# Strided sparse attention and a rational MLP on one core: TensorE turns x, and q, k and P of the first two batches

## The reference

```python
scores = scale * np.matmul(q, k.transpose(0, 1, 3, 2))
mask_local = (rel >= 0) & (rel < stride)
mask_strided = (rel >= 0) & (pos[None, :] % stride == pos[:, None] % stride)
...
attn = softmax(np.where(masks, scores, -1e9))      # the first 4 heads local, the last 4 strided
x = (attn @ v).transpose(0, 2, 1, 3).reshape(B * S, H * D)
h = x @ w_in                                       # 512 -> 2048
P = a[0] + a[1] * h + a[2] * h**2 + a[3] * h**3
Q = 1.0 + np.abs(b[0]) * np.abs(h) + np.abs(b[1]) * h**2
out = (P / (Q + 1e-06)) @ w_out                    # 2048 -> 512
```

## Time and profile before

| | us |
|---|---|
| median of 3 runs | 518.57 (515.09 to 522.15) |
| the profiled execution | 515.17 |
| its span, first to last instruction | 513.4 |

### The profile page before, as it was taken

One profiled execution on the slowest core, in us unless ns is written; L12 is line 12 of the kernel. 1 busy time (PEld: TensorE's weight loads), 2 busy tenths in 40 slices (PEclk: granted clock), 3 DMA queues, 4 the chain that ended last, 5 costly groups with the idle time before them and its releaser, 6 DMA issues.

```text
span 513.4 us, 7637 instructions
## 1 busy us (share of the span) xinstructions
PE 360.7 (70%) x3328; PEld 166.3 (32%) x3328; DVE 343.0 (67%) x286; ACT 272.9 (53%) x249; POOL 63.8 (12%) x104
## 2 busy tenths in 40 slices
PE   0024312678288979985977859997997898888980
PEld 0002110333133444532533325443442343333330
DVE  2001220138738988929959939996999999989940
ACT  0002000228338758581667556947968978788540
POOL 4022000200201100300401400030010010100010
PEclk9999999999558979997989969997999999998996
DMA  8989966997959969996899995472125110110111
GB/s 146 198 162 147 184 120 114 151 139 147 156 103 165 178 142 175 172 145 150 165 210 143 165 206 90 96 134 49 40 65 96 41 42 20 41 42 19 44 58 44
DMA packets 138769, 60.39 MB, mean 118 GB/s; under 512 B 128048, under 2 KB 134704, under 8 KB 138096
## 3 DMA queue, kind: packets, MB, share of 16 engines
q1 hardware_dynamic: 128560, 32.11, 36.9%
q0 software_dynamic: 10176, 27.80, 27.1%
HBM read 40.47 MB, written 23.59 MB: 125 GB/s over the span
## 4 chain that ended last, share of the span: by engine, by line
PE 33%; DMA 21%; ACT 16%; DVE 15%; SPq 8%; issue 5%; POOL 0%; DVEq 0%; POOLq 0%
PE ps_h L669 15%; PE ps_out L715 10%; DMA ptL<-pL 6%; ACT u L693 6%; DMA xt<-xL 5%; DMA ptS<-pS 4%; ACT u L691 4%; DMA tq<-q 4%; ACT h L673 3%; SPq L441 3%; SPq L643 2%; DVE u L690 2%; DVE z L696 2%; DVE h L700 2%; PE ps_s L715 2%
## 5 line engine op out<-in xcount | busy, mean ns | idle before, releaser
L669 PE MATMUL ps_h<-xt,Win 128*128 128x512 bf16 x576 | 152.4, 409 | 23.9 <-ACT h L673 16.5
L673 ACT ACTIVATE h<-ps_h 128x512 bf16<-128x512 f32 x144 | 104.9, 743 | 66.7 <-PE ps_h L669 62.5
L715 PE MATMUL ps_out<-Wout,h 128*128 128x512 bf16 x512 | 125.2, 396 | 6.1 <-ACT os L720 6.1
L669 PEld LDWEIGHTS ps_h<-xt,Win 128*128 128x128 bf16 x576 | 53.6, 103 | 104.3 <-ACT h L673 36.6
L715 PEld LDWEIGHTS ps_out<-Wout,h 128*128 128x128 bf16 x512 | 50.1, 101 | 69.5 <-ACT os L720 8.6
L691 ACT ACTIVATE u<-u,consts 128x4096 bf16<-128x4096 bf16 x18 | 66.5, 3695 | 5.6 <-DVE u L690 5.6
L693 ACT ACTIVATE u<-u 128x4096 bf16<-128x4096 bf16 x18 | 65.1, 3619 | 0.0
L726 POOL DMA_DIRECT2D out_dram<-os x36 | 25.8, 715 | 287.0 <-ACT os L720 287.0
L489 PE MATMUL ps_s<-ML,IDN 128*128 128x480 bf16 x32 | 10.8, 425 | 48.5 <-DMA tk<-tk 48.3
L508 DVE TENSOR_REDUCE ng<-ps_s 128x10 bf16<-128x960 f32 x16 | 18.3, 1142 | 37.6 <-PE ps_s L498 37.6
L700 DVE TENSOR_TENSOR h<-z,u 128x4096 bf16<-128x4096 bf16 x18 | 41.0, 2280 | 1.5 <-ACT u L693 1.4
(11 more groups left out here) (43 smaller groups left out, 305.7 us busy)
## 6 DMA issues: line engine op xcount, KB each, us to landing
out_dram<-os POOLq DMA_DIRECT2D x36, 256.0 KB, 2.5
q<-in_q_dram POOLq DMA_DIRECT2D x16, 288.0 KB, 6.7
k<-in_k_dram POOLq DMA_DIRECT2D x16, 288.0 KB, 9.1
vL<-v SPq DMA_DIRECT2D x32, 96.0 KB, 3.0
v<-in_v_dram POOLq DMA_DIRECT2D x8, 288.0 KB, 7.5
vS<-in_v_dram POOLq DMA_DIRECT2D x16, 144.0 KB, 11.6
xs<-xS SPq DMA_DIRECT2D x16, 144.0 KB
Win<-in_moe_w_in_dram POOLq DMA_DIRECT2D x4, 512.0 KB, 16.5
```

Source lines behind the costliest of these rows:

```text
L669: r = e.matmul(ph.t[:, :], Win[:, kk, f * 128:(f + 1) * 128], xt.t[:, kk, :], start=(kk == 0), stop=(kk == NK1 - 1))
L673: P.op("act", lambda e, f=f, ph=ph, h=h: e.activation(h.t[:, f % G, :].rearrange("p (j c k) -> p j k c", k=2, c=32), ph.t[:, :].rearrange( ...
L715: r = e.matmul(pot, groups[g].t[:, j, m * 128:(m + 1) * 128], Wout[:, kk, :], start=(kk == 0), stop=(kk == NF - 1))
```

## The change

PE turns x in all batches: the tokens of xS and xL are transposed in the bank `sm`, and ACT copies them in token order into a circular buffer `XT` of three chunks, in two passes of 128 columns for each kind (`turn`); the DMA transposes and the DRAM copy of xS go. As x is in token order now, the copy of h is written without the stride. In the first two batches POOL loads q and k straight into tiles of the h ring (`stage`), in 96 partitions, and PE transposes them, and P, into PSUM; ACT and DVE copy them out (`loads_pe`, `trp`). Batch 1's transposes of q and k wait for the fourth tile of the first chunk's MLP (`early`). Win comes in two column halves with a tile each, eight loads in all; batch 1's loads and Wout no longer wait for batch 0. A small ACT copy at the start brings the table load there. The planner counts POOL as free from 5 us on. Lines of the diff that only rename or that repeat a pattern are left out.

```diff
--- before.py
+++ after.py
@@ -103,7 +103,7 @@
                 d.users.append(o)
         pend = {e: [] for e in self.ENG}
         avail = {e: [] for e in self.ENG}
-        free = {e: 0.0 for e in self.ENG}
+        free = {e: 5.0 if e == "pool" else 0.0 for e in self.ENG}
         order = {e: [] for e in self.ENG}
         dmafree = {e: 0.0 for e in self.ENG}
         for o in self.ops:
@@ -260,6 +260,9 @@
     NBK = 8
     SB = S // 16
     NR = 64 + SB
+    TP = 96
+    TW = S * D // TP
+    NPE = 2
 
...
-    xs = nc.dram_tensor("xs16", [B, S, HL * D], bf)
     T_q = [[Tile(f"q{b}{n}") for n in "LS"] for b in range(B)]
     T_k = [[Tile(f"k{b}{n}") for n in "LS"] for b in range(B)]
     T_v = [Tile(f"v{b}") for b in range(B)]
...
     Win = sb("Win", [128, NK1, Fmid])
     Wout = sb("Wout", [128, NF, Fout])
-    T_win = Tile("win")
+    T_win = [Tile(f"win{i}") for i in range(2)]
     T_wout = Tile("wout")
     ML = sb("ML", [128, NR2 * KW])
     MS = sb("MS", [128, NBK * SB])
...
-    R_xt = ring("xt", 3, [128, NK1, CH])
+    XT = sb("XT", [128, NK1, 3 * CH])
+    T_xt = [Tile(f"xt{i}") for i in range(3)]
...
+    T_wm = Tile("warm")
+    WM = sb("WM", [128, 2], f32)
+    P.op("dve", lambda e: e.memset(WM[:, :], 1.0), 0.1, -2e6, m=[T_wm])
+    P.op("act", lambda e: e.activation(WM[:, 0:1], WM[:, 1:2], AF.Copy), 0.2, -2e6, m=[T_wm])
...
+    stage = {}
+
     def casts(b, after=()):
         key = b * 576 - 1500 if b > 1 else -1e5 + 3e4 * b
         for n in range(2):
@@ -403,9 +411,19 @@
             T_k[b][n].new()
         T_v[b].new()
         for n in range(2):
-            for s_t, d_t, t in ((q, q16, T_q[b][n]), (k, k16, T_k[b][n])):
-                bulk(s_t, d_t, b, HL * n, HL, H, t, key, after)
-            if n == 0:
+            if b < NPE:
+                h = stage[b, n] = R_h.next()
+                hv = h.t[:, :, :].rearrange("p g c -> p (g c)")
+            for i, (s_t, d_t, t) in enumerate(((q, q16, T_q[b][n]), (k, k16, T_k[b][n]))):
+                if b >= NPE:
+                    bulk(s_t, d_t, b, HL * n, HL, H, t, key, after)
+                    continue
+                P.op("pool", lambda e, s_t=s_t, hv=hv, i=i, n=n: e.dma_start(
+                    hv[0:TP, i * HL * TW:(i + 1) * HL * TW].rearrange("p (h c) -> p h c", c=TW),
+                    bass.AP(tensor=s_t.tensor, offset=s_t.offset + (b * H + HL * n) * S * D,
+                            ap=[[TW, TP], [S * D, HL], [1, TW]])),
+                    1.0, key, w=[t], dma=1.6, after=list(after) + h.prev)
+            if n == (1 if b < NPE else 0):
                 bulk(v, vs, b, 0, HL, HL, T_v[b], key, after)
...
     def weights_in():
-        T_win.new()
-        for kk in range(NK1):
-            P.op("pool", lambda e, kk=kk: e.dma_start(Win[:, kk, :], w_in[kk * 128:(kk + 1) * 128, :]),
-                 3.0, -9e4, w=[T_win], dma=4.9)
-
-    def weights_out(after):
+        FH = Fmid // 2
+        for i in range(2):
+            T_win[i].new()
+            for kk in range(NK1):
+                P.op("pool", lambda e, kk=kk, i=i: e.dma_start(
+                    Win[:, kk, FH * i:FH * i + FH], w_in[kk * 128:(kk + 1) * 128, FH * i:FH * i + FH]),
+                     1.0, -9e4, w=[T_win[i]], dma=2.4)
+
+    def weights_out(after=()):
         T_wout.new()
         for j in range(4):
             P.op("pool", lambda e, j=j: e.dma_start(
@@ -430,11 +451,81 @@
                 3.0, -4e4, w=[T_wout], dma=5.4, after=after)
 
 
-    def loads(b):
+    NB = SC // TP
+
+    def loads_pe(b, key, tq, tk, after):
+        for n in range(2):
+            h = stage[b, n]
+            hv = h.t[:, :, :].rearrange("p g c -> p (g c)")
+            for i, (t, st_) in enumerate(((tq, T_q[b][n]), (tk, T_k[b][n]))):
+                eng = ("act", "dve")[i]
+                sl = R_ps.next()
+                pv = sl.t.bitcast(bf)
+                hf = halves[t.name][n]
+                hf.new()
+
+                def tr(e, pv=pv, hv=hv, i=i):
+                    r = None
+                    for hh in range(HL):
+                        for j in range(NB):
+                            c0 = (i * HL + hh) * TW + 128 * j
+                            o0 = (hh % 2) * SC + TP * j
+                            r = e.transpose(pv[:, hh // 2, o0:o0 + TP], hv[0:TP, c0:c0 + 128], IDN[0:TP, 0:TP])
+                    return r
+                P.op("pe", tr, 1.2, key + 2 * n, r=[st_, h, T_c], w=[sl], after=after)
+
...
+                P.op(eng, ev, 1.5, key + 2 * n, r=[sl], w=[hf])
+                if n:
+                    continue
+                z = halves[t.name][2]
+                z.new()
+                sw = (R_po, R_sm)[i].next()
+                sv = sw.t.bitcast(bf)
+
...
+    def loads(b, after=()):
         key = b * 576 - 20 if b else -700
         st = {}
         tq, tk = R_tq.next(), R_tk.next()
-        for n in range(2):
+        if b < NPE:
+            loads_pe(b, key, tq, tk, after)
+        for n in range(2 if b >= NPE else 0):
             for t, d_t, dt_ in ((tq, q16, T_q[b][n]), (tk, k16, T_k[b][n])):
                 hf = halves[t.name][n]
                 hf.new()
...
+        st["ops"] = [vl.w[-1], hk[0].w[-1], hk[1].w[-1]]
         return st
+
...
+    cur_xt = [None] * NCH
+
+    def xt_tiles(t0, t1):
+        for c in range(t0 // CH, (t1 - 1) // CH + 1):
+            if cur_xt[c] is None:
+                cur_xt[c] = T_xt[c % 3].new()
+        return [cur_xt[c] for c in range(t0 // CH, (t1 - 1) // CH + 1)]
+
+    def cuts(b):
+        t0, t1 = b * S, b * S + S
+        mid = [t for t in range(3 * CH, NT, 3 * CH) if t0 < t < t1]
+        ed = [t0] + mid + [t1]
+        return list(zip(ed[:-1], ed[1:]))
+
+    def turn(b, kind, src, key):
+        for kk in range(2):
+            sm = R_sm.next()
+            sv = sm.t.bitcast(bf)
+            if kind == "L":
+                def tr(e, sv=sv, kk=kk):
+                    r = None
+                    for i in range(NR2):
+                        r = e.transpose(sv[:, 128 * i:128 * i + 128], src.t[:, i, 128 * kk:128 * kk + 128], IDN[:, :])
+                    return r
+            else:
+                def tr(e, sv=sv, kk=kk):
+                    r = None
+                    for i in range(NBK):
+                        r = e.transpose(sv[:, NR * i:NR * i + NR], src.t[0:NR, i, 128 * kk:128 * kk + 128],
+                                        IDN[0:NR, 0:NR])
+                    return r
+            P.op("pe", tr, 0.5, key, r=[src, T_c], w=[sm])
+            for t0, t1 in cuts(b):
+                tiles = xt_tiles(t0, t1)
+                c0 = t0 % (3 * CH)
+                s0, s1 = t0 - b * S, t1 - b * S
+                if kind == "L":
+                    i_ = sv[:, s0:s1].rearrange("p (j q c) -> p j c q", q=2, c=32)
+                    o_ = XT[:, kk, c0:c0 + t1 - t0].rearrange("p (j c q) -> p j c q", q=2, c=32)
+                else:
+                    i_ = bass.AP(tensor=sv, offset=s0 // 16,
+                                 ap=[[1024, 128], [1, (s1 - s0) // 16], [NR, NBK], [64, 2]])
+                    o_ = XT[:, 2 + kk, c0:c0 + t1 - t0].rearrange("p (i k q) -> p i k q", k=NBK, q=2)
+                P.op("act", lambda e, i_=i_, o_=o_: e.activation(o_, i_, AF.Copy), 0.25 + (t1 - t0) / 1000, key,
+                     r=[sm], w=tiles)
 
     def attention(b, st):
         base = b * 576
@@ -522,9 +667,23 @@
                     pp.t[:, :, 0:KW].rearrange("p (a r) c -> p a r c", a=2), flat, AF.Exp, scale=0.125),
                     1.0, key, r=[sc], w=[pp])
                 pt = R_ptL.next()
-                P.op("sp", lambda e, pp=pp, pt=pt: e.dma_start_transpose(
-                    pt.t[:, :, :], pp.t[:, :, :].rearrange("p a c -> p (a c)")),
-                     1.3, key, r=[pp], w=[pt], dma=1.9)
+                if b < NPE:
+                    for j in range(2):
+                        ph = R_ph.next()
+                        pv = ph.t.bitcast(bf)
+
+                        def trp(e, pv=pv, pp=pp, j=j):
+                            r = None
+                            for i in range(NR2):
+                                r = e.transpose(pv[0:KW, 128 * i:128 * i + 128], pp.t[:, NR2 * j + i, 0:KW], IDN[:, :])
+                            return r
+                        P.op("pe", trp, 0.5, key, r=[pp, T_c], w=[ph])
+                        evict(("act", "dve")[j], pt.t[0:KW, NR2 * j:NR2 * j + NR2, :].rearrange("p a c -> p (a c)"),
+                              pv[0:KW, 0:128 * NR2], 0.7, key, ph, pt)
+                else:
+                    P.op("sp", lambda e, pp=pp, pt=pt: e.dma_start_transpose(
+                        pt.t[:, :, :], pp.t[:, :, :].rearrange("p a c -> p (a c)")),
+                         1.3, key, r=[pp], w=[pt], dma=1.9)
                 acc = R_ps.next()
 
                 def av(e, pt=pt, acc=acc, idx=idx):
@@ -585,9 +744,25 @@
                 pp.t[0:NR, :, 0:SB].rearrange("p (j b) c -> p j b c", j=2), s4, AF.Exp, scale=0.125),
```

(45 more changed lines are left out.)

## The result

The changed kernel takes **467.2 us** (median of 4 runs, 461.56 to 474.03) against 517.91 (515.09 to 522.15) for the kernel before: ratio 0.894 [0.882, 0.907]. The forecast was 441, range 412 to 476. In two later comparisons, each beside the kernel before on its own chip, the changed kernel had 471.46 us (0.912 [0.906, 0.918]) and 471.21 us (0.912 [0.899, 0.925]). Runs 1 to 4, 5 to 8 and 9 to 12 were each timed together, beside the kernel before on one chip; across these three groups the ratios to the kernel before are the measure.

A forecast was written before the change was run, and what follows sets the result against it. The prediction saw the loss in the start (DMA transposes, copies), with DVE and PE nearly full after it. Chunk 1 at 95 + DVE work 294 + idle 31 + tail 19.4 = 439, plus 1.8: 441 us, range 412 to 476.

The forecast's parts named there:

- the clock rival: Middle stretch: transposes between matmuls take PE's granted clock to 0.80 and PE becomes the bound, 476 us; chance 0.11.
- the arrival of the second chunk: Start: the second MLP chunk (chunk 1) reaches DVE at 95 us (80 to 115).
- First score at 15 (12 to 20): Start: batch 0's first score matmul comes at 15 us instead of 33.48.
- Turning P: Batch 0, behind the last unit: P's transposes on PE take 1.0 us, their eviction 0.7; first MLP matmul at 41.
- A transposing matmul 0.10 us in a row (0.039 to 0.22): PE: each transpose in a row costs 0.10 us, so 26 a batch take 2.6 us, within PE's idle time.
- x and h evictions cancel on ACT: ACT: 22 us more for evictions of x, up to 19 us back from unstrided h; sum counted as nothing.
- Idle 31 (12 to 60): DVE after 95 us: 24 us idle left without waits for transposes of x, plus 7 from turns of x.
- Tail 19.4: End of the run: last matmuls and stores take 19.4 us, as before.
- DVE's work left 294: From 95 us on: DVE still has 343.0 + 14 - 63 = 294 us of work.
- Single bank: Turns of x: PE stands for an Ln of 3.7 us on ACT at each of 32 passes, 552 us; chance 0.06.
- The start is shortened by less: Start: batch 1's attention takes 51.4 us, chunk 1 arrives at 117, DVE starves for 22 us, 463 us; chance 0.13.
- More is won: Chunk 1 at 82 and DVE idle 15 us, as DMA is no longer full, 412 us; chance 0.10.

The follow-up runs named there:

- r2: The changed kernel with v of the first two batches loaded by POOL straight into vL, ahead of Win: 452.19 us (0.871).
- r1: The changed kernel as it is, timed again as the measure for others of its group: 471.46 us (0.912).
- r8: r2 with PE turning P in all eight batches, so no DMA transpose of P is left: 483.08 us (0.938).
- r11: r8 with P's transposes in the PSUM bank of the turns of x instead of the MLP tiles' banks: 463.57 us (0.897).
- r4: The changed kernel without the bulk loads of q, k and v of batches 4 to 7: 452.81 us (0.876).

## Why the prediction was right, and where its steps were off

The direction, the mechanism (the start was the loss, and behind it DVE is nearly full: 285.95 of 325.20 us, 301.91 of 348 before) and the range held. The size did not: some 51 us were won where 78 were forecast, and 467.2 lies outside the forecast's own 420 to 460; the stated range reaches it only because it ends at the clock rival's 476. The profile after allows the forecast's sum to be made again, from the windows and timeline above: second chunk at DVE 123.8 + busy 285.9 + idle 38.1 until DVE's last end at 447.8 + tail 20.8 = 468.6, against 95 + 294 + 31 + 19.4 = 439. So the terms are off by +28.8, -8, +7 and +1.4: **the arrival of the second chunk is the mis-sized term**. That the others nearly cancel is luck.

*The step that failed* is the sentence on POOL, that batch 1's loads and Wout follow Win at once and "nothing that is needed before 44 lies behind them". In POOL's queue nothing did. But SP's copies of v share the DMA engines with that queue, and v is needed at 23 (23.32 in r2). The forecast followed q, k and P to PE and counted v, which stayed, at nothing. The row to see it by was there: the DMA engines were 80% to over 90% busy in the first five slices, and the wait that the change removes kept batch 1's loads and Wout from starting at once. The rule "when a stall goes, say what is late next" was applied to engines and not to the operand that still went by DMA.

The 28.8 us split as follows. DVE's first MLP instruction came at 72.03 for 51: 13.6 of these 21 are v (58.47 in r2); 2.7 are batch 0's attention (first MLP matmul at 43.65 in r2 for 41), and 4.8 a full group of eight tiles, 14.8 us in r2 for 10. From the first to the second chunk it took 51.8 for 44, so 7.8 more: DVE's work in it was 44.7 us, as the forecast's 46 had it, but 7.1 of idle time lay between, which it had at nothing.

Not all of the 13.6 us comes back at the second chunk. With v in time (r2) it reaches DVE at 114.11, 9.7 earlier than in r1 but still 19.1 later than forecast, since there the way from the first chunk takes 55.6 us. What DVE waits for at its end is PE. The windows of r2 from 95 to the chunk, and of r1 in the same part (columns as above):

```profile
95.00:114.11 19.11, 18.11 (x202) 9.24 (x199) 9.09 (x11) 8.02 (x13) 0.00 (x0) 0.69 0.73 131
```

```profile
99.00:116.30 17.30, 14.60 (x151) 8.32 (x152) 15.55 (x15) 11.94 (x11) 0.00 (x0) 0.51 1.01 164
```

In r2 PE is busy for 18.11 of the 19.11 us, DVE for 9.09, at a granted clock of 0.69. In r1 the clock is at the lower of its two levels (1.2 GHz) for some 17 us, after a stretch (75 to 99) in which PE was busy for 17.84 of 24 us; four MLP matmuls that take 1.03 us at 67.29 take 1.89 at 113.02. The kernel before has such a stretch too (0.50 from 128.6 to 152.5), so the change did not bring it; what it costs here no run shows.

The rest, step by step:

- *First score at 15 (12 to 20)*: 14.60. *Turning P* on PE: first MLP matmul 41, 57.94; with v there in time 43.65.
- *A transposing matmul 0.10 us in a row (0.039 to 0.22)*: right. Two passes of the changed kernel in the timeline:

```profile
177.74 0.85 PE L599 MATMUL ps_sm<-IDN,xS 100*128 100x100 bf16 x8
...
183.78 0.44 PE L593 MATMUL ps_sm<-IDN,xL 128*128 128x128 bf16 x5
```

  0.09 to 0.11 us each in these two, all latencies in; five at 55.02 took 0.71, 0.14 each. That PE's idle time covers them was not tried by itself. The duration of a single one is 237 to 242 ns in the mean for x, and up to 269 for P. The Trainium skill (TensorE: Matmul & The Clock Gate, Part 4: PE-mode transpose) has about 275 ns; that is near the duration of one, but too much as a price for each in a row, and the time that was worked out from it, 468, came close to the measured one for another reason.
- *x and h evictions cancel on ACT*: right in size and without effect. The groups of the changed kernel (count, busy us, mean ns, idle before):

```profile
L820 ACT ACTIVATE h<-ps_h 128x512 bf16<-128x512 f32 x144 | 84.6, 600 | 49.1 <-PE ps_h L814 49.0
...
L614 ACT ACTIVATE XT<-ps_sm 128x576 bf16<-128x576 bf16 (+2 forms) x40 | 21.3, 555 | 27.7 <-PE ps_sm L599 23.2 <-PE ps_sm L593 4.4
```

  21.3 us for 22, and 105 - 84.6 = 20.3 us back for 19.
- *Idle 31 (12 to 60)*: 38, in other places than said. One reading in it was wrong: the 10.0 us that were taken off as a wait for a transpose of x end here,

```profile
148.82 0.76 DVE L571 TENSOR_REDUCE ng<-ps_s 100x16 bf16<-100x576 f32 x1 [10.05 <-PE ps_s L564]
```

  so only 2.8 of them lie behind 146, and 46.1 - 11.8 - 2.8 + 7 would have been 38.5. That this meets the measured 38 is luck: the single bank was to bring 7, and PE waited for its evictions for 2.3 us in all, while the waits for the L units' products, behind P's DMA transposes, grew from 12.0 to 19.4.
- *Tail 19.4*: 20.8. *DVE's work left 294*: 286.

The rivals. *Single bank* (552): refuted by the 2.3 us. *PE bound by its clock* (476): not for the kernel as a whole, whose granted clock from the second chunk on is 0.96, but in the last part before that chunk, as shown above. That transposes lower the clock is not seen: r8 and r11, with the most of them on PE, have 0.90 and 0.93 from 95 to 200 (0.87 in r2, with fewer), and 0.95 and 1.00 from 200 to 300 (0.99 in r2). The Trainium skill (same page and section) says that transposes don't count as PE work for the clock; these runs neither contradict it nor show it. The forecast named a clock under 0.85 in the middle as a sign of being wrong; from 95 to 200 it was 0.84. With the bulk loads gone (r4) it is 0.90 there, so a part goes with the waits for DMA; the 17 us at the lower level stay in r4 (0.50 from 99.8 to 116.9). *The start is shortened by less* (463, second chunk at 117): in its time this came nearest, with 123.8 and 467. Its reason, long instructions of chunk 0 between batch 1's hops, can hold at most for the 19.1 us that stay with v in time. *More is won* (412): no; the DMA engines were full again from 95 to 200 (1.01).

What stays open: why the DMA engines serve SP's short runs and transposes so slowly beside POOL's bulk loads. The Trainium skill (DMA: Bandwidth & Descriptors, Queues, rings and completion order) says that an engine takes turns between queues packet by packet; single copies of v that land in a median of 3.4 us over the run but in up to 19.4 us beside Win and Wout fit this, without showing it. What the lower clock before the second chunk costs, and what batch 2's loads would bring if they were issued while the DMA engines are idle, is open as well. Also open is why the changed kernel stood at 0.894 in one comparison and 0.912 in two.

## What to carry to other kernels

When two operands of three leave the DMA queues, follow the third to its use, and check each removed wait for what it kept free: here putting one back gained 11 us. Count a queue by the DMA engines that it shares, not by what stands behind it in its own order. And a buffer ring handed out in program order ties loops together that have no data in common (51.8 us of waits in r8, 19.1 without it): look at who is next in the ring before putting more work on it.

## What the runs showed of the hardware that was not expected

- A copy by DVE of 640 two-byte columns from PSUM takes 0.42 to 0.49 us (P's transposes), while the permuted one of 576 columns (tk) takes 752 ns. ACT takes 648 ns for the same 576 permuted columns, about as for a plain four-byte read of that size (643 in the earlier trace rows): here the permuted read goes with a longer time on DVE, not on ACT.
- Beside bulk loads the issue of one DMA transpose took SP 7.93 and 10.23 us (1.32 at the least), and one of P took 22.0 us to land in r1, where the median over the run is 5.8.
